# One kernel for attention with memory and two feed-forward stages: the order of the early attention steps, of the steps with tiles, and the engine that splits x

## The chip, the cores and the metric

The kernel runs on one core of one Trainium2 chip. The metric is the device time of one execution in microseconds (us). The engines are called as in the profile: PE is TensorE (PEld its weight loads), DVE is VectorE, ACT is ScalarE, POOL is GpSimd, SP is the engine that issues the DMAs.

## The reference

```python
def _attn_ref(q, k, v, M_prev, z_prev, beta):      # B, H, S, D = 4, 8, 576, 64
    scores = scale * np.matmul(q, k.transpose(0, 1, 3, 2))     # then a causal mask
    a = np.exp(scores - scores.max(-1, keepdims=True))
    a /= a.sum(-1, keepdims=True) + 1e-09
    local = np.matmul(a, v)
    q_p = np.where(q > 0, q, np.exp(q) - 1.0) + 1.0
    mem_out = (q_p @ M_prev) / (q_p @ z_prev + 1e-06)
    return g * mem_out + (1 - g) * local                       # g = sigmoid(beta) by head
def _moe_ref(x, w_in, w_out, g_ln):                # x: 2304 x 512, d_ff 1024
    h = x @ w_in
    solu = h * softmax(h)
    ln = (solu - mean) / np.sqrt(var + 1e-06) * g_ln
    return ln @ w_out
def _moe2_ref(x, w_gate, w_val, w_out):            # d_ff 1536
    return (sigmoid(x @ w_gate) * (x @ w_val)) @ w_out
```

## The kernel before, in words

All is fp32. The big products are made from high and low halves: an fp32r copy of a matrix (hi, an ACT cast) and what it leaves (lo, a subtraction), and three products hi*hi, hi*lo, lo*hi for each one.

Every engine has an order of its own, written out by hand, and the engines meet by semaphores. There are 16 pairs of heads (g=0 to 15) and 18 tiles of 128 tokens (t=0 to 17). In the early steps g=0 to 4 (`early_step`) there is attention alone. From g=5 (`step(g, t)`, t = g - 5) to g=16 a step holds the attention of pair g and the first feed-forward stage of tile t, and the output product of tile t-1. Then tiles 12 to 17 follow, and then the last stage.

Attention of one pair: PE makes the scores in four batches, `scores(g, 0)` to `scores(g, 3)`; the first three hold units 0 and 1, 2 and 3, 4 and 5, the last one unit 6. They are S0 to S3 in what follows. For each unit DVE takes the negated maximum and writes the scores out (`unit_max`, L905), and ACT makes the exponents and their sums (`exp_tile`, L588). DVE scales them by one over the sum (`normalize`, L929), in three batches. The units of S0, S1, S2 take turns in three banks of PSUM, so `scores(g, 2)` waits for the maximum of unit 2 and `scores(g, 3)` for that of unit 4:

```python
                elif n == 2:
                    pe.wait_ge(max_ok, NU * g + 3)
                else:
                    pe.wait_ge(max_ok, NU * g + 5)
```

In the next step PE turns P by seven groups of transposes (`turn_p`, L1349) through two banks, and each group is copied out to pT (`keep_pt`, L595 on ACT, L949 on DVE in steps with tiles); group n waits for copy n-2. In the step behind that one `weighted` makes the weighted values of P and v, with the memory's part turned in ahead (L1357, L1361): a main part over 512 tokens in o_bk and a tail over 64. ACT's `keep_x` copies both to xT (L602); tile by tile xT is the input of the feed-forward stage. `memory` (L1405) multiplies the features of q (`feature_relu`, `feature_exp` on ACT, `feature` on DVE, L913, called phi) with the memory, and DVE scales its result (`scale_memory`, L934 to L941).

Feed-forward of a tile: ACT casts x_hi (`moe_x`, L616), `split_x` makes x_lo (POOL, L546), PE makes 24 hidden products (`moe_hidden`, L1420), DVE and ACT make softmax and mean (`moe_max`, `moe_exp`, `moe_rows`, `moe_square`), POOL one over the deviation (`rstd`, L551), DVE the normalized rows (`moe_norm`, L1001). In the next step PE transposes them (`moe_transpose`, L1430), ACT casts ln_hi (`moe_ln`, L633), DVE makes ln_lo (`moe_ln_low`, L1008), and PE makes 24 output products (`moe_out`, L1444). The result is turned (`moe_out_t`, L1451) and stored back to xT (`moe_store_x`, L988).

x_hi of a tile is cast at the end of the step before, if all pairs that it needs are stored by then. The tiles for which this is not so are called OWN: t=0 and t=4. Their x_hi is cast in their own step, behind `keep_both`:

```python
        OWN = [t for t in range(PAIRS + 1 - M0) if HP * (((t + 1) * P - 1) // S + 1) > t + M0 - 2]
```

In the early steps the weights are split too, in between: w1 by `split_w1` (ACT L606, DVE L953), w2 by `split_w2` (ACT L611, DVE L958).

## Time and profile before

| | |
|---|---|
| runs | 845.44, 845.45, 846.02 us; median 845.45 |
| the profiled execution | 845.53 us, with a span of 843.5 us from the first to the last instruction |
| busy | PE 816.5, PEld 686.0, DVE 601.1, ACT 466.3, POOL 39.0 us |
| granted TensorE clock, mean | 0.995 |
| early steps g=1 to 4 | 11.73 to 64.17 us |
| steps with tiles, t=0 to 11 | 64.17 to 337.95 us |
| tiles 12 to 17, then the last stage | from 337.95 us |

Times in the rows are microseconds from the span's start. Matmuls are pipelined, and the busy time of PE takes in their overlap, so idle time of PE in the rows is a little less than the time lost: a row with "[0.40 <-DVE negmax L905]" says that PE had no instruction in flight for 0.40 us, and what ended that.

### The profile page before, as it was taken

Reading aid. Unit: us, or ns where it says so; the run is one execution under the profiler, and the core shown is the slowest. Engines: PE = TensorE matmul, PEld = TensorE weight load, DVE = VectorE, ACT = ScalarE, POOL = GpSimd, SP = SyncE. Lnnn points to the kernel's source line nnn. Section 1 sums busy time; section 2 is a strip of 40 time slices with the busy share of each in tenths; the row PEclk is TensorE's granted clock in tenths of the full one; section 3 lists DMA queues with packets and bytes.
Section 4 is the critical chain, followed back from the end, with each engine's and each line's share of the span. In section 5 each row is a group of like instructions: output and inputs, shape, how many; then the busy total and the mean of one; then the engine's idle time right before and its main releaser. Section 6 shows DMA issues by size and latency. Waiting matters only on the chain.

```text
span 843.5 us, 15401 instructions
## 1 busy us (share of the span) xinstructions
PE 816.5 (97%) x5704; PEld 686.0 (81%) x5704; DVE 601.1 (71%) x1447; ACT 466.3 (55%) x965; POOL 39.0 (5%) x47
## 2 busy tenths in 40 slices
PE   5888999999999999999999999999999999999997
PEld 3555777777777777878889999999999999999996
DVE  6988877777777775588565777687676678666653
ACT  6987666666566663364444444574444465444442
POOL 1000000000000001111000000000000000000000
PEclk8999999999999999999999999999999999999999
DMA  7353011111111000100224111103111113111002
GB/s 219 91 171 88 18 53 54 53 54 54 47 44 54 26 18 15 51 1 1 75 54 148 51 51 51 51 26 125 50 51 51 51 27 125 51 51 50 26 1 76
DMA packets 67034, 49.51 MB, mean 59 GB/s; under 512 B 9360, under 2 KB 57488, under 8 KB 66960
## 3 DMA queue, kind: packets, MB, share of 16 engines
q1 hardware_dynamic: 66960, 48.53, 19.3%
q8 instruction: 46, 0.75, 0.4%
q14 instruction: 28, 0.23, 0.1%
HBM read 43.79 MB, written 4.72 MB: 58 GB/s over the span
## 4 chain that ended last, share of the span: by engine, by line
PE 90%; DVE 5%; issue 2%; ACT 2%; SPq 1%; DMA 1%; POOL 0%; DVEq 0%; ACTq 0%
PE tt_bk L1554 10%; PE tt_bk L1552 10%; PE tt_bk L1553 10%; PE m_bk L1420 10%; PE s_bk L1444 7%; PE tt_bk L1349 5%; PE s_bk L1290 4%; PE o_bk L1357 4%; PE o_bk L1444 4%; PE s_bk L1604 3%; PE s_bk L1605 3%; PE s_bk L1603 3%; PE m_bk L1604 2%; PE m_bk L1605 2%; PE m_bk L1603 2%
## 5 line engine op out<-in xcount | busy, mean ns | idle before, releaser
L1554 PE MATMUL tt_bk<-xc_hi,wc_lo 128*128 128x384 f32 x476 | 160.0, 336 | 0.0
L1552 PE MATMUL tt_bk<-xc_hi,wc_hi 128*128 128x384 f32 x476 | 159.9, 336 | 0.0
L1553 PE MATMUL tt_bk<-xc_lo,wc_hi 128*128 128x384 f32 x476 | 159.8, 336 | 0.0
L588 ACT ACTIVATE p_nat<-p_nat,negmax 128x512 f32<-128x512 f32 (+2 forms) x144 | 83.0, 579 | 53.3 <-DVE negmax L905 53.3
L1133 DVE TENSOR_TENSOR wc_lo<-wc_raw,wc_hi 128x768 fp32r<-128x768 f32 x72 | 78.3, 1088 | 32.0 <-ACT wc_hi L653 32.0
L1552 PEld LDWEIGHTS tt_bk<-xc_hi,wc_hi 128*128 128x128 f32 x476 | 89.4, 188 | 6.1
L1553 PEld LDWEIGHTS tt_bk<-xc_lo,wc_hi 128*128 128x128 f32 x476 | 89.4, 188 | 6.1
L1554 PEld LDWEIGHTS tt_bk<-xc_hi,wc_lo 128*128 128x128 f32 x476 | 89.4, 188 | 0.0
L905 DVE CUSTOM_DVE_ANT_0 p_nat<-s_bk,mask 128x384 f32<-128x384 f32 (+2 forms) x124 | 54.9, 489 | 19.4 <-PE s_bk L1290 18.9
L653 ACT CAST wc_hi<-wc_raw 128x768 fp32r<-128x768 f32 x72 | 64.5, 946 | 3.1 <-DVE wc_raw L1127 3.1
L1349 PE MATMUL tt_bk<-ident,p_nat 128*128 128x128 f32 x400 | 56.6, 277 | 7.6 <-ACT pT L595 7.4
L595 ACT COPY pT<-tt_bk 128x512 f32<-128x512 f32 (+1 forms) x87 | 45.7, 552 | 31.9 <-PE tt_bk L1349 30.3
L1349 PEld LDWEIGHTS tt_bk<-ident,p_nat 128*128 128x128 f32 x400 | 46.7, 142 | 20.2 <-issue 13.4
L1290 PE MATMUL s_bk<-qkT 64*64 64x512 f32 (+3 forms) x496 | 47.7, 473 | 9.4 <-DMA qkT<-in_k 4.9
L1420 PE MATMUL m_bk<-w_hi,x_hi 128*128 128x512 f32 x120 | 50.5, 421 | 1.2 <-issue 1.2
L929 DVE TENSOR_SCALAR p_nat<-p_nat,c_loc 128x512 f32<-128x512 f32 (+2 forms) x144 | 50.1, 405 | 1.7
L690 ACT ACTIVATE gv_b<-tt_bk 128x384 f32<-128x384 f32 x34 | 16.7, 492 | 55.3 <-PE tt_bk L1554 55.3
L1420 PE MATMUL m_bk<-w_hi,x_lo 128*128 128x512 f32 x120 | 47.1, 392 | 0.0
L1420 PE MATMUL m_bk<-w_lo,x_hi 128*128 128x512 f32 x120 | 46.8, 390 | 0.0
L1149 DVE TENSOR_TENSOR c_u<-c_u,tt_bk 128x384 f32<-128x384 f32 x34 | 18.8, 553 | 37.4 <-ACT c_u L685 37.3
L700 ACT CAST gv_hia<-gv_a 128x384 fp32r<-128x384 f32 x36 | 18.5, 513 | 39.4 <-DVE gv_a L1164 39.4
L675 ACT ACTIVATE gv_a<-c_p 128x384 f32<-128x384 f32 x36 | 18.9, 526 | 36.3 <-DVE c_p L1144 36.3
(215 smaller groups left out, 1781.1 us busy)
## 6 DMA issues: line engine op xcount, KB each, us to landing
wc_raw<-in_moe_w_val SPq DMA_DIRECT2D x36, 256.0 KB, 3.0
wc_raw<-in_moe_w_gate SPq DMA_DIRECT2D x36, 256.0 KB, 3.4
qkT<-in_q SPq DMA_DIRECT2D x16, 288.0 KB, 2.8
qkT<-in_k SPq DMA_DIRECT2D x16, 288.0 KB, 3.2
v_raw<-in_v SPq DMA_DIRECT2D x16, 256.0 KB, 2.7
out<-o_sb SPq DMA_DIRECT2D x15, 256.0 KB, 2.5
w_raw<-in_moe_w_out SPq DMA_DIRECT2D x12, 256.0 KB, 4.5
turned<-in_k SPq DMA_DIRECT2D x32, 72.0 KB, 2.5
```

The lines of the kernel that those rows point to most:

```text
L588: nc.scalar.activation(p_tile(g, tile), p_tile(g, tile), ACT.Exp, bias=negmax[:, n:n + 1], scale=-1.0, accum_out=den[:, n:n + 1]).then_inc ...
L653: nc.scalar.copy(wc_hi[n % 2][:, k, :, :], wc_raw[n % NR][:, r, :, :]).then_inc(wc_hi_ok, 1)
L905: last = nc.vector.tensor_tensor_reduce(out=to, in0=s_tile(g, tile), in1=m, scale=-SCALE, scalar=3.0e38, op0=ALU.add, op1=ALU.min, accum_o ...
L929: nc.vector.tensor_scalar(p, p, c_loc[:, t:t + 1], None, ALU.mult).then_inc(p_ok, 1)
L1133: nc.vector.tensor_tensor(wc_lo[n % 2][:, k, :, :], wc_raw[n % NR][:, r, :, :], wc_hi[n % 2][:, k, :, :].bitcast(F32), ALU.subtract).then_ ...
L1290: last = mm(s_tile(g, tile)[c * D:c * D + D, :], qkT[r, g % 2, 0, a:a + D], qkT[r, g % 2, 1, 0:keys(tile)], start=True, stop=True, skip_gr ...
L1349: last = nc.tensor.transpose(bank[:, c * P:(c + 1) * P], p_nat[g % 2][:, p_at[tile] + j * P:p_at[tile] + (j + 1) * P], ident[:, :])
L1420: last = mm(h_banks(even)[:, n, :], x[:, b, :], w[:, b, c], start=m % (3 * DC) == 0, stop=m % (3 * DC) == 3 * DC - 1)
L1444: last = mm(y_bank(tail), ln[:, f * P:(f + 1) * P], w[:, f, :], start=m == 0, stop=m == 3 * FB - 1)
L1552: mm(o, hi[:, k, c, :], xc_hi[:, j, c, :], start=start and c == 0, stop=False, skip_group_check=True)
L1553: mm(o, hi[:, k, c, :], xc_lo[:, j, c, :], start=False, stop=False, skip_group_check=True)
L1554: last = mm(o, lo[:, k, c, :], xc_hi[:, j, c, :], start=False, stop=c == 1, skip_group_check=True)
```

## The change

1. In early steps PE makes the main part of the weighted values, then S1, then the tail; the memory's products stand behind transposes 2; S2 comes ahead of them. ACT takes copy n early: copy 0 between the two parts of `keep_x`, copies 1 and 2 ahead of the exponents of unit 2, and copies 3 to 6 ahead of exponents 4 to 8. DVE normalizes the first batch ahead of units 4 and 5, and takes unit 6 between the two parts of the memory's scaling; `feature` is last but for the splits of weights.
2. In steps with tiles PE makes S1 between the main part and the tail of the weighted values (t=1 excepted), and S2 always straight behind the memory's products; before it stood there for OWN tiles alone and else behind 12 of the hidden products. In the last of these steps (g=16) y is turned behind the weighted values, and ln ahead of them; ACT's and DVE's shares in ln_hi and ln_lo move ahead there too.
3. x_lo of tiles 0 to 12, but for t=4, is made on DVE and no longer on POOL: for t=0 behind units 2 and 3, for the others at the end of the step before.
4. In the first tile behind these steps ln_hi is cast ahead of `moe_square(t + 2)`, and ln_lo is made ahead of `moe_var(t + 2)`.

```diff
@@ gpsimd
-            def step(g):
-                if g >= M0:
-                    rstd(g - M0)
-                if g >= M0 - 1:
-                    split_x(g - M0 + 1)
-
-            for g in range(PAIRS + 1):
-                step(g)
+            def step(g, t):
+                if t and t in OWN:
+                    split_x(t)
+                rstd(t)
+
+            for g in range(M0, PAIRS + 1):
+                step(g, g - M0)
@@ scalar, early_step
                 exp_tile(g, 0)
                 exp_tile(g, 1)
                 if g > 1:
-                    keep_both(g - 2)
+                    keep_x(g - 2, 0)
                 if g:
                     keep_pt(g - 1, 0)
+                if g > 1:
+                    keep_x(g - 2, 1)
+                if g:
                     keep_pt(g - 1, 1)
-                for n in range(2, 6):
+                    keep_pt(g - 1, 2)
+                exp_tile(g, 2)
+                exp_tile(g, 3)
+                if g:
+                    for n in range(3, NF):
+                        keep_pt(g - 1, n)
+                for n in range(4, 6):
                     exp_tile(g, n)
-                if g:
-                    keep_pt(g - 1, 2)
-                    keep_pt(g - 1, 3)
                 for c in W1_HI_MID.get(g, ()):
                     split_w1(c)
                 for f in W2_HI_MID.get(g, ()):
                     split_w2(f)
                 exp_tile(g, 6)
                 exp_tile(g, 7)
-                if g:
-                    keep_pt(g - 1, 4)
-                    keep_pt(g - 1, 5)
-                    keep_pt(g - 1, 6)
@@ scalar, step
-                if t > 1 and g < PAIRS:
+                if t > 1:
                     moe_ln(t - 1)
                 keep_both(g - 2)
-                if t == 1 or g == PAIRS:
+                if t == 1:
                     moe_ln(t - 1)
@@ scalar, behind the steps
             moe_y(t, True)
+            moe_ln(t + 1)
             moe_square(t + 2)
             for i in range(t + 1, TILES):
                 even = (i - t) % 2 == 1
-                moe_ln(i)
+                if i > t + 1:
+                    moe_ln(i)
@@ vector
+            def split_x(t):
+                dve.wait_ge(x_hi_ok, t + 1)
+                nc.vector.tensor_tensor(x_lo[:, :, :], xT[:, :, bass.ds(t * P, P)],
+                                        x_hi[:, :, :].bitcast(F32), ALU.subtract).then_inc(x_lo_ok, 1)
@@ vector, early_step
                 unit_max(g, 2)
                 unit_max(g, 3)
+                normalize(g, 0)
+                unit_max(g, 4)
+                unit_max(g, 5)
                 if g:
                     scale_memory(g - 1, 0)
+                unit_max(g, 6)
+                if g:
                     scale_memory(g - 1, 1)
                     for c in W1_LO_MEM.get(g, ()):
                         split_w1(c)
-                unit_max(g, 4)
-                unit_max(g, 5)
                 feature(g)
...
-                unit_max(g, 6)
-                normalize(g, 0)
@@ vector, step
-                if t > 1 and g < PAIRS:
+                if t:
                     moe_ln_low(t - 1)
                 if t != 1:
                     normalize(g - 1, 2)
                 if g == PAIRS:
                     moe_store_x(t - 2)
-                if t == 1 or g == PAIRS:
-                    moe_ln_low(t - 1)
                 if g < PAIRS:
                     unit_max(g, 2)
                     unit_max(g, 3)
+                if t == 0:
+                    split_x(t)
...
                 moe_var(t)
                 moe_norm(t)
+                if t + 1 not in OWN:
+                    split_x(t + 1)
@@ vector, behind the steps
             moe_stats(t + 2)
-            low_xc(0, B21)
+            moe_ln_low(t + 1)
             moe_var(t + 2)
             moe_norm(t + 2, False)
+            low_xc(0, B21)
             for i in range(t + 1, TILES):
                 even = (i - t) % 2 == 1
-                moe_ln_low(i)
+                if i > t + 1:
+                    moe_ln_low(i)
@@ tensor, early_step (weighted is cut into weighted_main and weighted_tail)
                 scores(g, 0)
                 if g > 1:
-                    weighted(g - 2)
+                    weighted_main(g - 2)
                 scores(g, 1)
+                if g > 1:
+                    weighted_tail(g - 2)
                 if g:
                     turn_p(g - 1, 0)
                     turn_p(g - 1, 1)
-                    memory(g - 1, None)
                 scores(g, 2)
                 if g:
-                    for n in range(2, 5):
-                        turn_p(g - 1, n)
+                    turn_p(g - 1, 2)
+                    memory(g - 1, None)
+                    turn_p(g - 1, 3)
+                    turn_p(g - 1, 4)
                 scores(g, 3)
@@ tensor, step
                 if g < PAIRS:
                     scores(g, 0)
-                if g == PAIRS:
-                    pe.wait_ge(u_ok, t)
-                    weighted(g - 2)
-                if t > 1:
+                if 1 < t and g < PAIRS:
                     moe_out_t(t - 2)
...
+                weighted_main(g - 2)
+                if t == 1:
+                    weighted_tail(g - 2)
+                    moe_transpose(t - 1)
                 if g < PAIRS:
-                    weighted(g - 2)
-                if t == 1:
-                    moe_transpose(t - 1)
+                    wait(pe, yt_ok, t - 1)
+                    scores(g, 1)
+                if t != 1:
+                    weighted_tail(g - 2)
+                if g == PAIRS:
+                    moe_out_t(t - 2)
                 wait(pe, yt_ok, t - 1)
+                memory(g - 1, t)
                 if g < PAIRS:
-                    scores(g, 1)
-                memory(g - 1, t)
-                if t in OWN and g < PAIRS:
                     scores(g, 2)
                 pe.wait_ge(x_ok, 2 * (g - 1))
                 wait(pe, u_ok, t)
                 moe_hidden(t, 0, 12)
-                if t not in OWN and g < PAIRS:
-                    scores(g, 2)
```

## Rows read from the trace of the kernel before

**Rows 1.** Who PE waited for, whole span: us in total, times, longest.

```profile
PE tt_bk L1349 <- ACT pT L595: 7.4, 9, 1.2
...
PE s_bk L1290 <- DVE negmax L905: 2.4, 4, 0.9
...
PE tt_bk L1405 <- DVE ln_lo L1008: 1.5, 1, 1.5
```

**Rows 2.** Busy time by stretch: steps g=1 to 4, then t=3 and t=4.

```profile
11.73:24.38 12.65, 10.24 (x105) 5.70 (x106) 11.92 (x45) 10.96 (x31) 0.00 (x0) 0.73 0.64 210
24.38:37.97 13.59, 11.16 (x155) 7.17 (x155) 12.48 (x43) 12.75 (x33) 0.00 (x0) 1.00 0.30 87
37.97:50.79 12.82, 11.09 (x155) 7.15 (x155) 11.67 (x43) 10.70 (x29) 0.00 (x0) 1.00 0.33 98
50.79:64.17 13.38, 11.08 (x155) 7.17 (x154) 11.67 (x43) 11.54 (x31) 0.00 (x0) 1.00 0.77 232
...
131.05:154.21 23.16, 23.16 (x215) 17.33 (x214) 17.18 (x55) 14.13 (x35) 1.63 (x2) 1.00 0.17 47
154.21:177.68 23.47, 23.07 (x215) 17.43 (x215) 17.10 (x55) 15.33 (x36) 2.33 (x3) 1.00 0.18 49
```

**Rows 3.** Timeline of PE in t=3 (start, us, instruction): S2, first transpose.

```profile
141.52 0.66 PE L1290 MATMUL s_bk<-qkT 64*64 64x256 f32 x8
...
143.60 0.60 PE L1349 MATMUL tt_bk<-ident,p_nat 128*128 128x128 f32 x4
```

**Rows 4.** Timeline of DVE in t=3: unit 0, four normalized tiles, unit 2.

```profile
132.31 0.69 DVE L905 CUSTOM_DVE_ANT_0 p_nat<-s_bk,mask 128x512 f32<-128x512 f32 x1 [1.31 <-PE s_bk L1290]
...
134.54 1.14 DVE L929 TENSOR_SCALAR p_nat<-p_nat,c_loc 128x384 f32<-128x384 f32 x4
...
138.20 0.56 DVE L905 CUSTOM_DVE_ANT_0 p_nat<-s_bk,mask 128x384 f32<-128x384 f32 x1
```

**Rows 5.** Timeline of PE in t=4: S2, first hidden product, first transpose.

```profile
162.20 0.66 PE L1290 MATMUL s_bk<-qkT 64*64 64x256 f32 x8 [0.40 <-DVE negmax L905]
162.82 0.47 PE L1420 MATMUL m_bk<-w_hi,x_hi 128*128 128x512 f32 x1
...
167.01 0.93 PE L1349 MATMUL tt_bk<-ident,p_nat 128*128 128x128 f32 x7
```

**Rows 6.** Timelines of ACT and POOL in t=4: keep_x of the tail, x_hi, x_lo.

```profile
160.25 0.21 ACT L602 COPY xT<-m_bk 128x64 f32<-128x64 f32 x1
160.55 0.62 ACT L616 CAST x_hi<-xT 128x512 fp32r<-128x512 f32 x1
...
161.25 1.29 POOL L546 TENSOR_TENSOR x_lo<-xT,x_hi 128x512 fp32r<-128x512 f32 x1 [8.30 <-ACT x_hi L616]
```

**Rows 7.** Timelines of ACT in g=1 (w1_hi) and of DVE at g=2's start.

```profile
21.25 1.05 ACT L606 CAST w_hi<-xT 128x1024 fp32r<-128x1024 f32 x1
...
25.64 0.69 DVE L905 CUSTOM_DVE_ANT_0 p_nat<-s_bk,mask 128x512 f32<-128x512 f32 x1 [0.20 <-PE s_bk L1290]
```

**Rows 8.** Timelines of ACT and PE in t=0: x_hi, first hidden product.

```profile
70.53 0.62 ACT L616 CAST x_hi<-xT 128x512 fp32r<-128x512 f32 x1
...
72.69 0.47 PE L1420 MATMUL m_bk<-w_hi,x_hi 128*128 128x512 f32 x1 [1.17 <-issue]
```

**Rows 9.** Timeline of DVE in t=1: four normalized tiles.

```profile
88.06 2.16 DVE L929 TENSOR_SCALAR p_nat<-p_nat,c_loc 128x384 f32<-128x384 f32 x4
```

**Rows 10.** Timelines of PE and DVE in t=11: ln turned, memory's products, stored x.

```profile
320.62 1.04 PE L1430 MATMUL tt_bk<-ident,u_moe 128*128 128x128 f32 x8
323.27 0.81 PE L1405 MATMUL tt_bk<-mz,phi 64*64 64x66 f32 x40 [1.61 <-issue]
...
320.83 0.69 DVE L988 TENSOR_SCALAR xT<-s_bk 128x512 f32<-128x512 f32 x1 [0.29 <-PE s_bk L1451]
```

**Rows 11.** Timelines of DVE and PE at the first tile behind the steps: ln_lo, output product.

```profile
365.71 1.28 DVE L1008 TENSOR_TENSOR ln_lo<-tt_bk,ln_hi 128x512 fp32r<-128x512 f32 x2
...
367.05 0.50 PE L1444 MATMUL o_bk<-w_hi,ln_hi 128*128 128x512 f32 x1 [0.70 <-DVE ln_lo L1008]
```

More of the change, by code:

```diff
@@ L1362, in turn_memory, with weighted_main @@
                    is_transpose=True, skip_group_check=True)
-            def weighted(h):
+            def weighted_main(h):
                 wait(pe, x_ok, 2 * h)
@@ L1381, in weighted, with weighted_tail @@
                 last.then_inc(o_ready, 1)
+            def weighted_tail(h):
                 for j in range(ST):
@@ L1385, in weighted @@
                 last.then_inc(o_ready, 1)
+            def weighted(h):
+                weighted_main(h)
+                weighted_tail(h)
             def memory(g, t):
```

## The prediction

> **What bounds the kernel now.** I first read who TensorE (PE) waits for [rows 1, 8, 10]. Apart from some 7 us of start-up loads, its own idle time is about 16 us of 843.5, all before 370 us. It lies where the change works: 7.4 us at transposes of P that wait for ScalarE's (ACT's) copies, 2.4 us at scores that wait for VectorE's (DVE's) maxima, and the single waits of 1.6, 1.5 and 1.2 us at the memory's products of steps t=11 and t=1 and at the first hidden product of t=0. Behind 370 us PE works nearly without a gap, and the diff moves nothing there. So the sum is made in six places before that.
>
> Next, the work per step [rows 2]. In the early steps g=1 to 4 DVE is busy 11.92 of 12.65, 12.48 of 13.59, 11.67 of 12.82 and 11.67 of 13.38 us: it is nearly the bound, with 4.70 us without work in all. ACT has 10.96, 12.75, 10.70 and 11.54, PE some 11. In a step with tiles the picture turns over: t=3 lasts 23.16 us and PE is busy in all of it, DVE in 17.18. Such a step is PE's own work. It can only be shortened by taking work from PE, and can be lengthened by any new wait.
>
> **The third batch of scores, t=2 to 10.** S2 (units 4 and 5) waits until DVE has taken the maximum of unit 2. In t=3, the pattern of all but one of these steps, S2 stands in the middle of the hidden products, at 141.52, and never waits; the first transpose of P is at 143.60 [rows 3]. The step began at 131.05, so that is 12.55 us in. DVE is idle until the first scores come at 132.31 and then works without a gap: two maxima, the stored x, four normalized tiles, the low half of ln, three normalized tiles, and only then unit 2 from 138.20 to 138.90, 7.85 us in [rows 4]. The change leaves this order of DVE as it is for t=2 to 10. But it puts S2 straight behind the memory's products for all t. PE gets there some 7.6 us in (memory's products at 6.83 before, 0.7 long, and one more change of shape of 0.1, since the weighted tail now stands behind S1). So S2 waits.
>
> The trace has this very order already: t=4 is an OWN tile, and S2 stood behind the memory's products there. It waits 0.40 us for negmax, starts at 162.20, 7.99 us in, and the first transpose comes at 167.01, 12.80 us in [rows 5]. The order saves PE two changes of shape (S2 and 18 hidden products take 4.81 us together, against 5.03 for 12 products' tail, S2 and 6 more), but the wait costs more: +0.25 us to the transpose, +0.31 by the whole step, 23.47 against 23.16 [rows 2]. I take 0.28 for each of t=2, 3 and 5 to 10: **+2.2 us**. Moving S1 ahead of the weighted tail makes S1 ready 0.7 us sooner for DVE, but DVE comes to unit 2 only when its other work is done, and gains nothing by it. Bounds: if the wait were gone and the saved changes of shape alone were left, -0.15 per step, -1.2 us; if the full 0.40 came on top of an unchanged length, +3.2.
>
> **t=4 itself.** Its x_hi is cast behind keep_x of the tail, and that waits for the weighted tail, which now comes behind S1, 0.9 to 1.0 us later. In the trace keep_x of the tail starts at 160.25, x_hi at 160.55, the low half on GpSimd (POOL) at 161.25, 1.29 long to 162.54 [rows 6], and the first hidden product starts right behind S2 at 162.82 [rows 5]. There is no slack but 0.15. POOL keeps this one, so the hidden products start at about 163.7: **+0.85** (0 if something else gives, 1.0 at most).
>
> **Early steps.** The edits take DVE's wait for S1 (about 0.45 in each step) and PE's waits at the transposes away: copies 2 to 6 are taken before exponents they stood behind. With S2 and the maxima that follow moved up, DVE's idle time shrinks to 0.2 to 0.7 us in a step, waiting for S3. Against that ACT's splits of w1 and w2 now stand behind copies 3 to 6 and two exponents. For g=1 I follow the queue: unit 2's maximum ends at 18.3, S2 is at 18.5, copy 2 at 19.7 to 20.2, S3 at 21.1, transposes 5 and 6 at 21.8 and 22.4, copy 6 is done at 23.3, two exponents (0.99 the pair) at 24.3, and the cast of w1_hi block 0, which was at 21.25, ends at 25.25. DVE, which subtracts from it and started the next step at 25.64 [rows 7], is ready for it at 24.1, waits 1.3 us and starts the next step at 26.5: +0.9. g=2 has 0.7 us of idle DVE instead of 1.1 and next starts at 40.0 where it was 39.2; g=3 0.2 instead of 1.15, at 51.7 where it was 52.05; g=4 0.3 and another 0.9 of waiting for w2_hi, together 1.2 instead of 1.7, at 64.7 where it was 65.44. ACT has the same casts and exponents before x_hi of t=0 and less idle time, but its queue is longer behind copy 6; by the same count x_hi still ends at 71.1, as before. What comes there is the swap of engines: POOL took 1.6 us from the cast to the first hidden product at 72.69 [rows 8], DVE about 0.9 (a half of ln, 128x512, takes 0.6 [rows 11]). So hidden at 72.0: **-0.7**. DVE is blocked at split_x(0) for about 1.5 us, with memory scaling, unit 4 and unit 6 behind it; unit 4 is then ready at 2.6 us behind the first hidden product, S3 needs it at 2.9. That cover is 0.3 us thin; without it the step loses what is missing. Bounds: all of DVE's 4.70 us gone, -4.7; ACT's queue 1.5 us later at x_hi, +0.8.
>
> **t=1.** DVE now waits for x_hi and subtracts (about 1.2 us) ahead of normalizing. In the trace four such tiles took 2.16 us there, while POOL subtracted too, against 1.14 in t=3 [rows 4, 9]. That 1.0 comes back, so low ln is 0.2 later, and S2 behind the memory's products costs or saves 0.1: **-0.1**, within 0.4.
>
> The Trainium skill (SBUF — State Buffer, Who interferes with whom) says that the port pair which DVE and GpSimd share is an exclusive lock, held for a whole instruction. The trace agrees, with the 2.16 us. By that rule alone nine more subtractions off POOL should bring time; in t=2 to 10 they lie in DVE's 1.31 us of idle time before the first scores [rows 4], so by rule and row alike they bring nothing there.
>
> **t=11.** PE transposed y and then ln at 320.62, and the memory's products waited until 323.27 for low ln [rows 10]. Now ln's transpose comes first at 316.7 and low ln is ready at 319.8. But y's transpose, behind the weighted values, ends at 321.6, and the wait for yt_ok behind it takes DVE's store, 0.7 from transpose to start and 0.6 long [rows 10]: 322.5. **-0.75** (the full 1.6 at best).
>
> **The first steps behind.** PE waited 0.70 us at 367.05 for low ln, which DVE did at 365.71 [rows 11]. It now stands 2.2 us earlier on DVE, and the later maxima move up with it: **-0.75**; 0 if the next tile's low ln takes the wait back.
>
> GpSimd's freed queue, keep_x in two parts and qrelu's wait for phi (now at DVE's end, some 0.1 before ACT asks) I cost at nothing; if phi is late, ACT's exponent 8 is, and 0.2 a step go.
>
> **Sum.** 2.2 + 0.85 - 0.7 - 0.1 - 0.75 - 0.75 = +0.75. The profiled execution took 845.53, 2.0 beside its span, and the median is 845.45; both are one number here: **846.3 us**, no measurable change (within 0.2%, 843.8 to 847.1).
>
> **Rivals.** (A) The early steps run as smoothly as the edits allow: DVE's idle time goes nearly whole, since the casts of w1 and w2 are in time. From -0.7 to -4 there, 842.9 us: faster. It decides if the cast of w1_hi block 0 ends by about 24.1. For it: ACT and PE have slack in [rows 2]; against it: the casts' new place. (B) The wait at S2 doesn't come, DVE being ahead: -1.2 instead of +2.2, also about 842.9. Against it stands t=4's row. (C) The ends of ACT's and DVE's queues get late: x_hi(0) 1.5 us late, and split_x(0) holds unit 4 so that S3, the copies and the maxima of t=0 slip another 0.8. 848.6: slower. It decides once unit 4's maximum is over 0.3 us late. For it: DVE's queue was free to go on there and now stops. (D) The steps with tiles hide everything and the early gains end in the wait for x_hi: nothing changes, 845.5; that lies in my band.
>
> **Chances.** The forecast with D 0.62; A 0.13 and B 0.06 make faster 0.19; C 0.19. The range of 8 in 10 takes in most of A and of C: 843.0 to 848.3. The likeliest case by itself is 845.2 to 847.4.
>
> **What would show it.** S2 of every step 2 to 10 waits about 0.4 us for negmax, and each lasts about 23.45; t=4 about 24.3; the first hidden product of t=0 is near 72.0; DVE waits for w_hi near 24 to 25 us; the waits at t=11 and 367 shrink to about 1 and 0. If S2 does not wait, or DVE's idle time in g=1 to 4 falls below 1.5 us in all, I am wrong on the fast side; if unit 4 of t=0 is late, on the slow side.

## The result and the profile after

The changed kernel takes **854.86 us**, the median of five runs (852.29 to 856.19), against 845.45 before (845.37 to 846.02): ratio 1.0105, 95% interval 1.0094 to 1.0117. It is slower by 1.0%, clear of the noise, and far outside the forecast's range (843.0 to 848.3). The profiled execution took 854.86 us with a span of 853.1, against 845.53 and 843.5.

The first view is the busy time by stretch of the changed kernel. The stretches are those of [rows 2] with t=0 added (fifth row), each from one S0 to the next: g=1 to 4, t=0, t=3, t=4. A row has the stretch and its length, then the busy time (and number of instructions) of PE, PEld, DVE, ACT and POOL, then TensorE's granted clock as a share of full speed, the DMA engines' busy share and their GB/s.

```profile
11.10:24.29 13.19, 10.19 (x106) 6.31 (x106) 10.74 (x45) 8.55 (x24) 0.00 (x0) 0.74 0.59 198
24.29:38.02 13.73, 11.34 (x154) 7.25 (x155) 11.34 (x42) 12.94 (x33) 0.00 (x0) 1.00 0.28 81
38.02:51.09 13.07, 11.32 (x155) 7.27 (x155) 12.33 (x43) 11.19 (x31) 0.00 (x0) 1.00 0.29 85
51.09:68.16 17.07, 12.04 (x155) 7.87 (x155) 11.69 (x43) 10.40 (x30) 0.00 (x0) 0.95 0.67 196
68.16:91.28 23.12, 19.47 (x180) 12.77 (x179) 18.46 (x53) 18.78 (x48) 0.00 (x0) 0.89 0.28 78
139.31:162.74 23.43, 23.40 (x216) 17.40 (x215) 17.60 (x56) 14.23 (x35) 0.55 (x1) 1.00 0.16 46
162.74:187.31 24.57, 23.41 (x215) 17.39 (x214) 17.12 (x56) 15.23 (x36) 1.82 (x2) 1.00 0.16 47
```

Start with the lengths. g=4 takes 17.07 us where [rows 2] has 13.38, and t=0 takes 23.12 where it took 19.04 (64.17 to 83.21). These two stages hold 7.8 of the 9.6 us that the span grew. The steps with tiles are as forecast: 23.43 against 23.16 in t=3, 24.57 against 23.47 in t=4. The whole account against the kernel before, from PE's rows, with t=10 ending at its last product:

| stage | longer by, us | forecast |
|---|---|---|
| start, 11.10 for 11.73 | -0.6 | |
| g=1 to 3 | +0.9 | in the early steps' -0.7 |
| g=4 | +3.7 | in the early steps' -0.7 |
| t=0 | +4.1 | in the early steps' -0.7 |
| t=1 | 0.0 | -0.1 |
| eight steps t=2, 3, 5 to 10 | +2.0 | +2.2 |
| t=4 | +1.1 | +0.85 |
| t=11 | -0.6 | -0.75 |
| first tiles behind | 0.0 | -0.75 |
| last product to the span's end | -1.0 | not named |
| sum | +9.6 | +0.75 |

The start and g=1 are no firm numbers. In the eighteen other profiles g=1 begins between 10.80 and 11.93 us, and it lasts 11.75 to 13.56 us in four kernels that make it in the same way (w2_late, gap_filled, cast_late and hi_first, below). g=2 and g=3 agree to 0.01 us in these four.

The second view is who PE waited for, whole span, as in [rows 1]: us in total, times, longest.

```profile
PE s_bk L1303 <- DVE negmax L908: 7.9, 11, 1.5
PE s_bk L1335 <- DMA turned<-in_k: 4.5, 1, 4.5
...
PE m_bk L1439 <- issue: 1.9, 1, 1.9
...
PE m_bk L1439 <- POOL x_lo L546: 1.1, 1, 1.1
PE tt_bk L1362 <- ACT pT L594: 1.0, 2, 0.6
```

The waits for ACT's copies are gone, 1.0 us instead of 7.4, which is what the early edits do. In their place stand 7.9 us for maxima, where [rows 1] has 2.4, and a single wait of 4.5 us for a DMA that the kernel before doesn't have at all. The timeline of PE around g=4's end and t=0 shows where (start, us, instruction):

```profile
60.28 0.99 PE L1362 MATMUL tt_bk<-ident,p_nat 128*128 128x128 f32 x7
65.79 0.46 PE L1335 MATMUL s_bk<-qkT 64*64 64x288 f32 x2 [4.52 <-DMA turned<-in_k]
...
76.58 0.66 PE L1303 MATMUL s_bk<-qkT 64*64 64x256 f32 x8 [1.06 <-DVE negmax L908]
79.14 0.47 PE L1439 MATMUL m_bk<-w_hi,x_hi 128*128 128x512 f32 x1 [1.90 <-issue]
...
80.27 0.63 PE L1439 MATMUL m_bk<-w_lo,x_hi 128*128 128x512 f32 x1
80.69 0.63 PE L1439 MATMUL m_bk<-w_hi,x_lo 128*128 128x512 f32 x1
```

S3 of g=4 stands for 4.52 us until `turned`, the small turned copy of k that S3 multiplies with, has landed. Then t=0 waits twice, ahead of S2 and of the hidden products. The first hidden product is at 79.14, 10.98 us into the step; in [rows 8] it is at 72.69, 8.52 in. And from the fifth product on one follows the other after 0.43 us, not 0.23. The view by stretch shows TensorE's clock behind either wait:

```profile
65.79:70.00 4.21, 4.21 (x24) 1.92 (x25) 2.19 (x6) 2.32 (x7) 0.00 (x0) 0.59 0.42 105
...
79.14:83.65 4.51, 4.51 (x12) 3.20 (x12) 4.32 (x15) 3.08 (x12) 0.00 (x0) 0.62 0.00 0
```

Behind the stall seven transposes took 1.75 us for the 0.99 ahead of it, and S0 1.85 for 1.09 in the kernel before, and the first 12 hidden products took 4.51 us where the kernel before takes 2.91. By these rows about 3 of the 7.8 us are the lower clock (an estimate: 0.8 and 0.8 and 1.6).

Why `turned` is late is read from DVE's and SP's timelines, first DVE, then SP's issues, both of the changed kernel:

```profile
51.68 1.22 DVE L956 TENSOR_TENSOR w_lo<-xT,w_hi 128x1024 fp32r<-128x1024 f32 x1
```

```profile
52.92 4.58 SPq L476 DMA_DIRECT2D xT<-in_moe_w_out  x8
57.67 0.33 SPq L417 DMA_DIRECT2D qkT<-in_q  x1
58.04 0.43 SPq L420 DMA_DIRECT2D qkT<-in_k  x1
58.57 0.47 SPq L433 DMA_DIRECT2D turned<-in_q  x1
59.09 0.62 SPq L435 DMA_DIRECT2D turned<-in_k  x1
59.75 0.60 SPq L433 DMA_DIRECT2D turned<-in_q  x1
60.39 0.60 SPq L435 DMA_DIRECT2D turned<-in_k  x1
```

The last block of w1's low half is made at 51.68. SP waits for it (`w1_lo_ok`) before it loads w2, eight transfers of 256 KB whose issue takes 4.58 us, and `turned` for S3 stands behind them on SP's queue. In the kernel before the same rows read like this:

```profile
47.04 1.21 DVE L953 TENSOR_TENSOR w_lo<-xT,w_hi 128x1024 fp32r<-128x1024 f32 x1
```

```profile
48.28 3.66 SPq L476 DMA_DIRECT2D xT<-in_moe_w_out  x8
...
55.17 1.30 SPq L435 DMA_DIRECT2D turned<-in_k  x1
```

So the block is 4.6 us later, the w2 loads 4.6 later, and the last `turned` load is issued 5.2 later. The DMA view has 5.3 us from issue to landing for it, 6.0 in the kernel before. There it landed at 61.2, and S3 began at 61.29: the queue had no slack. PE's wait ends 14 us behind the block that caused it.

### The profile page after: what moved, and what is told of

It is laid out like the page before. It is cut to its first block, busy times and chain, and to the rows that moved or that the text cites. A ratio compares the mean times of both kernels' runs of the same rounds, so it can differ in the third digit from the quotient of the medians.

```text
span 853.1 us, 15409 instructions
## 1 busy us (share of the span) xinstructions
PE 822.5 (96%) x5704; PEld 688.9 (81%) x5704; DVE 604.5 (71%) x1459; ACT 467.2 (55%) x965; POOL 20.7 (2%) x35
## 4 chain that ended last, share of the span: by engine, by line
PE 89%; DVE 4%; ACT 3%; issue 2%; DMA 1%; SPq 1%; POOL 0%; DVEq 0%; ACTq 0%
PE tt_bk L1576 10%; PE tt_bk L1574 10%; PE tt_bk L1575 10%; PE m_bk L1439 10%; PE s_bk L1463 7%; PE tt_bk L1362 5%; PE o_bk L1463 4%; PE s_bk L1303 3%; PE o_bk L1370 3%; PE s_bk L1626 3%; PE s_bk L1627 3%; PE s_bk L1625 3%; PE m_bk L1626 2%; PE m_bk L1627 2%; PE s_bk L1439 2%; PE m_bk L1625 2%
## 5 line engine op out<-in xcount | busy, mean ns | idle before, releaser
L1303 PEld LDWEIGHTS s_bk<-qkT 64*64 64x64 f32 x496 | 15.6, 136 | 32.3 <-issue 15.5
```

Source lines behind the costliest of these rows:

```text
L1303: last = mm(s_tile(g, tile)[c * D:c * D + D, :], qkT[r, g % 2, 0, a:a + D], qkT[r, g % 2, 1, 0:keys(tile)], start=True, stop=True, skip_gr ...
```

## The experiments

Each median stands beside the kernel before on the same chip, which read 845.28 to 845.6 us in all five groups of runs. "The early steps" are g=1 to 4. All of them compute the reference. Diffs are shortened to the lines that tell the edit.

**early_back**: the changed kernel, `early_step` of ACT, DVE and PE as before.

```diff
-  early_step as changed (scalar, vector, tensor)
+  early_step as before
```

> The early steps g=0 to 4 as they were before, on PE, ACT and DVE; the steps with tiles and what follows as changed. Theory Q (a queue): the 9.4 us come almost all from the early steps, where DVE's low half of w1 block 3 came 4.6 us later, SP's loads of w2 and the small loads of turned q and k behind them went out 4.6 us later, and S3 of g=4 waited 4.5 us for turned; what is left is the 0.26 us in each of eight steps with tiles, 1.1 in t=4, less 0.8 in t=11 and some 0.5 in t=0: 847.3 us, 846.8 to 848. Rival R (the steps with tiles cost most, through the swap of engines or the granted clock): over 850.

846.07 us (ratio 1.0008, 0.9998 to 1.0017). Nearly the whole loss, 8.8 us, goes with the three early orders. It is below the expected 846.8 to 848: t=0 takes 18.34 us, 0.70 less than before, which is the gain that the prediction named for it.

**early_only**: the kernel before with the changed `early_step` of the three engines.

> The kernel before with the changed early steps alone. Theory Q: S3 of g=4 waits 4 to 5 us for turned, the clock falls behind it, and the time is 852.5 to 854. Rival R: within 2 us of 845.45.

852.36 us (1.0077, 1.0058 to 1.0095), with the wait for `turned` 3.7 us long. So 7.0 us of the loss need nothing of the rest of the change.

**w2_late** and **c3_early**: two ways to take `turned` from behind the late w2 loads.

```diff
 w2_late, SP
-               if g == 3: wait w1_lo_ok; load w2       # ahead of all loads of the next step
+               if g == 4: wait w1_lo_ok; load w2       # behind load_turned(4)
 c3_early, DVE in g=3
                 unit_max(g, 2); unit_max(g, 3)
+                split_w1(3)
...
                 scale_memory(g - 1, 1)
-                split_w1(3)
```

> The changed kernel, but SP issues the eight loads of w2 behind the loads of turned q and k for g=4 and no longer ahead of all loads of that step. Theory Q: the wait of 4.5 us at S3 of g=4 goes, and with it the stretches at a granted clock of 0.5 to 0.6 in the 15 us behind it (2.3 us): 847.5 to 849. Rival A (ACT's queue, whose casts of w2 stand behind copies 3 to 6, is what is late, and turned only shows it first): at most 1 us better than the changed kernel, or worse, since w2 lands later: 853.5 or more.

> The changed kernel, but DVE makes the low half of w1 block 3 straight behind unit 3's maximum in g=3, some 4 us sooner, as early as before; the queue of SP is as it was. Theory Q: w2 goes out at about 48.5 us, turned for g=4 at about 53.5, no wait at S3: 847.5 to 849. Rival A: 853 or more.

849.14 us (1.0046) and 850.97 us (1.0060). The wait at S3 is gone in both, and 3.9 to 5.7 us with it; both medians lie above the expected 847.5 to 849, c3_early's by 2 us. What is left against early_back, 3 to 5 us, is in t=0, which takes 24.2 us in both profiles against 18.34. Some of that is the edit's own: w2_late issues the load of v behind w2's, and PE waits 0.45 us for v at t=0's start. Most of it is the gap ahead of the hidden products. There the profile of w2_late shows, in windows from the memory's products to the first hidden product and then over the first 12 of them:

```profile
69.23:73.86 4.63, 1.48 (x53) 0.91 (x49) 3.40 (x15) 4.60 (x13) 0.00 (x0) 0.91 0.29 74
73.86:79.25 5.39, 5.39 (x13) 3.81 (x13) 4.57 (x15) 3.96 (x13) 0.00 (x0) 0.50 0.00 0
```

PE is busy 1.48 of 4.63 us, then works without a gap at a granted clock of 0.50, the lower of its two levels (1.2 GHz of 2.4). The 12 products take 5.39 us; in the kernel before they take 2.91 at a clock of 1.00.

**gap_filled** asks whether that clock follows from the gap. It is w2_late with 12 products in the gap whose result nobody uses.

```diff
   memory(g - 1, t)
+  if t == 0: fill(5)      # w1_hi by w1_hi into a bank that is free
   scores(g, 2)
+  if t == 0: fill(7)
```

> The changed kernel with the w2 loads behind turned(4) (849.14 us), and in t=0 TensorE makes products that nobody uses while it would wait: five of 128x128 by 128x512 behind the memory's products, seven behind S2. They fill the 1.25 and 1.9 us of waiting and delay nothing that was waited for. Theory 1 (the granted clock falls because of this gap): the 12 hidden products take 2.9 instead of 5.4 us and t=1 begins 2.5 us earlier, 846.5 us. Theory 2 (the low clock comes by itself): 849.1 us or a little more.

847.99 us (1.0027, 1.0016 to 1.0039). The same two windows:

```profile
69.67:74.63 4.96, 4.64 (x65) 3.01 (x61) 3.71 (x17) 4.93 (x14) 0.00 (x0) 1.00 0.26 70
74.63:77.54 2.91, 2.91 (x12) 2.14 (x13) 2.80 (x11) 1.49 (x7) 0.00 (x0) 1.00 0.00 0
```

The gap filled, the clock stays at 1.00 and the 12 products take 2.91 us. In the profiles PE's useless work saves 2.5 us at these products. The medians differ by 1.15, with overlapping intervals, and both kernels spread over 2.5 to 2.9 us, the slower executions at the lower mean clock (w2_late 848.21 us at 0.994 to 850.73 at 0.989, gap_filled 846.23 at 0.998 to 849.11 at 0.994); in which stretch the clock was low in the executions without a profile isn't known. The gap isn't enough by itself, though: early_only has 1.42 of 4.65 us busy there and a clock of 1.00 behind it. Its low clock is at the step's start, 0.78 over the 6.98 us ahead of that gap, behind the wait for `turned`.

**cast_late** (w2_late, two of the three w2 casts at g=4's end moved into t=0) and **hi_first** (w2_late, in t=0 the products that need x_hi alone first).

```diff
-        W2_HI_TILE, W2_HI_END = {5: (5, 6)}, {4: (2, 3, 4), 5: (7,)}
+        W2_HI_TILE, W2_HI_END = {5: (3, 4, 5, 6)}, {4: (2,), 5: (7,)}    # block numbers by step
```

> The changed kernel with the w2 loads behind turned(4), and of the three w2 casts that ScalarE makes at the end of g=4, two moved into t=0 behind the feature relu. Theory 1 (ScalarE's longer queue delays keep_x and x_hi of t=0, the gap of some 3 us at S2 and the first hidden product follows from it, and the granted clock falls to 1.2 GHz behind that gap): x_hi 1.2 us earlier, first hidden product at about 72.6 instead of 73.9, the first 12 hidden products 2.93 us instead of 5.39, t=1 begins at about 83.5 instead of 87.1, 845.6 us against 849.14. Theory 2 (VectorE's late maximum of unit 2 sets it; the casts don't matter): S2 still at 71.3 and the products still at 73.9, 849 us. Theory 3 (the gap shrinks, but the clock falls all the same): 847.9 us.

> The changed kernel with the w2 loads behind turned(4), and in t=0 the eight hidden products of the first bank that need x_hi alone are made first, the four with x_lo behind them. Nothing else moves. Theory 1 (the gap between S2 and the hidden products, then the clock): the first hidden product 1.1 us earlier, at 72.8, and with the shorter gap the 12 products take 2.93 to 4 us: 845.6 to 848 us against 849.14. Theory 2 (the low clock does not hang on this gap): -1.1 us alone, 848.0 us. Theory 3 (x_lo isn't what the hidden products wait for): no change, 849.1 us.

847.87 us (1.0029) and 847.27 us (1.0028). In cast_late the first hidden product is 2.72 us behind the memory's products instead of 4.63, and the clock stays at 1.00. But it gave some back: two late casts cost 0.9 us at the transposes, and the wait for v is 1.12 us here. Its median is the 847.9 of the third theory, but by luck: that theory has the clock fall. hi_first took 0.9 us off the gap, with the clock at 0.63 behind it; its profile is 1.9 us shorter in t=0 than w2_late's, and 1.3 shorter in g=1, which the edit doesn't touch.

**early_act_back** and **early_dve_back**: the changed kernel with one engine's early order taken back.

> The changed kernel with ScalarE's order of the early steps as before; PE's and VectorE's stay changed. Theory 1 (ScalarE's order isn't what made the stall at S3 of g=4; copies 2 to 6 late again cost PE its 0.9 us a step): the stall stays, 855 to 857 us. Theory 2 (ScalarE's order made x_hi of t=0 late and that is most of the loss): 851 us.

> The changed kernel with VectorE's order of the early steps as before; PE's and ScalarE's stay changed. Theory 1 (VectorE's order made w1_lo block 3 late, 51.7 instead of 47.0 us, and with it the w2 loads and turned): the stall of 4.5 us at S3 of g=4 is gone, 850.4 us or less against 854.86. Theory 2 (PE's or ScalarE's order made it late): 854 us.

848.74 us (1.0050, 1.0037 to 1.0064) and 861.64 us (1.0202). Neither came out as its first theory had it. Taking ACT's order back removes 6.1 us of the loss. DVE's old order beside the other two new ones is far worse, with 17.8 us of waits for maxima: PE's and ACT's new orders need DVE's. With ACT's order back the wait for `turned` is still 3.6 us, but t=0 takes 19.06 us, as long as before, and g=1 to 3 take 37.94 us where they took 39.06. The reason is in ACT's and DVE's timelines of t=0's start, here in one list. First the changed kernel, S0 at 68.16:

```profile
67.62 1.12 ACT L594 COPY pT<-tt_bk 128x512 f32<-128x512 f32 x2 [5.55 <-PE tt_bk L1362]
...
69.64 1.32 ACT L610 ACTIVATE w_hi<-xT,g_col 128x512 fp32r<-128x512 f32 x2
...
70.38 1.42 DVE L961 SCALAR_TENSOR_TENSOR w_lo<-xT,g_col,w_hi 128x512 fp32r<-128x512 f32 x2 [1.42 <-ACT w_hi L610]
71.71 0.69 DVE L908 CUSTOM_DVE_ANT_0 p_nat<-s_bk,mask 128x512 f32<-128x512 f32 x1
...
71.85 0.67 ACT L575 ACTIVATE qrelu<-qkT 128x576 f32<-128x576 f32 x1
...
77.70 0.62 ACT L615 CAST x_hi<-xT 128x512 fp32r<-128x512 f32 x1
```

and with ACT's order back, S0 at 66.00:

```profile
60.77 1.33 ACT L610 ACTIVATE w_hi<-xT,g_col 128x512 fp32r<-128x512 f32 x2 [0.90 <-DMA xT<-in_moe_w_out]
...
67.06 0.68 ACT L575 ACTIVATE qrelu<-qkT 128x576 f32<-128x576 f32 x1 [0.47 <-DMA qkT<-in_q]
...
68.20 0.68 DVE L906 CUSTOM_DVE_ANT_0 p_nat<-s_bk,mask 128x512 f32<-128x512 f32 x1
...
73.10 0.62 ACT L615 CAST x_hi<-xT 128x512 fp32r<-128x512 f32 x1
```

and in the kernel before, S0 at 64.17:

```profile
64.66 0.69 ACT L576 ACTIVATE qrelu<-qkT 128x576 f32<-128x576 f32 x1
```

In the new ACT order four exponents and the two w2 casts stand behind copies 3 to 6, which wait for PE's transposes, and these for S3. ACT stands idle for 5.55 us and then has that work left when t=0 begins. It comes to the relu of q 3.69 us behind S0, where it was 0.49, and from there to x_hi the work is the same, 5.85 us for 5.87. ACT isn't idle once between 67.62 and x_hi at 77.70: its own queue sets x_hi. w2_late, without the stall, has nearly the same (relu 3.59 us behind S0, x_hi 9.45), so this is the order and not the late `turned`. By another way DVE is late too: its low halves wait 1.42 us for the casts, and unit 0 of t=0 starts 3.55 us behind S0, not 2.2, and 1.27 in the kernel before. That delays unit 2, and so S2.

**early_mended** and **early_two**: can the early orders pay once this is mended? Both have the steps with tiles of order_back, below, the weighted values in one piece, and w1_lo block 3 early. early_mended keeps all three new orders, with the edits of cast_late and hi_first; early_two has ACT's old order.

> The kernel with the order back, but with the changed early steps, mended where they went wrong: w1_lo block 3 ahead in g=3, two w2 casts moved into t=0, in t=0 the products that need x_hi alone first, and the weighted values in one piece in the early steps too. Theory 1 (the changed order of the early steps gains nothing by itself; its waits for DVE and the casts only stand elsewhere): 843 to 844 us, no better than the kernel with the order back. Theory 2 (once the two late queues are mended its gain of 0.7 us or more shows): 842.3 us or less.

> The kernel with the order back (843.05 us), with PE's and VectorE's changed orders in the early steps (the weighted values in one piece), ScalarE's order of before, and w1_lo block 3 right behind unit 3 in g=3 so that the w2 loads are in time. Theory 1 (ScalarE's changed order made the loss; PE's and VectorE's alone gain, as S0 of g=1 to S0 of g=4 took 37.9 us against 39.1 before): 841 to 842 us. Theory 2 (the gain is given back at t=0 all the same): 843 us.

845.79 us (843.21 to 847.59) and 844.17 us (842.51 to 845.63), against 843.05 for order_back. In early_mended the early steps are shorter (S0 of g=1 to S0 of t=0: 50.9 us, 52.4 before; 1.0 of the 1.5 is g=1, which isn't firm), and it is given back in t=0, 21.1 us for 19.0: S2 waits 2.06 us there for a maximum, and the clock behind the gap is 0.62. In early_two t=0 is in order, 18.6 us, but g=3 took 14.95 us for 12.82, with a wait of 1.8 us for a maximum ahead of S2 and a mean granted clock of 0.89. Neither expectation of a gain came true. The runs also spread by 3 to 4 us, where order_back's lie within 1, and the slowest have the lowest mean clock (early_two 842.51 us at 0.998, 845.63 at 0.992).

**s2_back**, **s1_back** and **order_back** take the steps with tiles apart, all three with the early steps as before.

```diff
 s1_back, PE:  weighted_main(g - 2)
-              scores(g, 1); weighted_tail(g - 2)
+              weighted_tail(g - 2); scores(g, 1)
 s2_back, PE:  memory(g - 1, t)
-              scores(g, 2)
               moe_hidden(t, 0, 12)
+              scores(g, 2)          # OWN tiles keep theirs
 order_back = both
```

> The changed kernel with the early steps as before and, in the steps with tiles that are not OWN, S2 once more behind 12 hidden products. Only the place of S2 is taken back beside the early steps; S1 still parts the weighted values. Theory 1 (the wait of S2 for unit 2's maximum makes the longer steps): the eight steps t=2, 3, 5 to 10 fall from 23.42 to 23.16 us, 844.0 us in all against 846.07 with S2 ahead of the hidden products. Theory 2 (S1 between the two parts of the weighted values is what costs, by its changes of shape): the steps stay at 23.4, 846 us.

> As the kernel with S2 back, and S1 behind the weighted tail too, so that of the change only x_lo on VectorE, the order of t=11 and the first tile behind the steps are left. Theory 1: t=4 falls from 24.5 to 23.47 us, the other steps keep 23.16 or lose 0.05: 842.9 to 843.5 us, faster than before by 1.9 to 2.5 us. Theory 2 (what is left of the change gains nothing, its gains are given back behind 435 us): 845.3 us, the time before.

> The changed kernel with the early steps as before and, in the steps with tiles, S1 behind the weighted tail again; S2 stays straight behind the memory's products in every step. Theory 1 (the prediction's: S2 waits for unit 2's maximum, +0.28 us in each of eight steps): 845.3 us against the 843.05 of the kernel with both back. Theory 2 (S1 between the two parts is what costs; S2's place costs nothing): 843.0 us, steps of 23.1 to 23.2.

| | S2 | S1 | median, us | step t=3, us | step t=4, us |
|---|---|---|---|---|---|
| early_back | ahead | parts | 846.07 | 23.41 | 24.60 |
| s2_back | back | parts | 846.52 | 23.48 | 24.59 |
| s1_back | ahead | back | 845.11 | 23.50 | 23.48 |
| order_back | back | back | **843.05** | 23.17 | 23.47 |

Here is t=3 of s1_back, S2 straight behind the memory's products and S1 at its old place:

```profile
138.13 0.76 PE L1421 MATMUL tt_bk<-mz,phi 64*64 64x66 f32 x40
139.28 0.66 PE L1300 MATMUL s_bk<-qkT 64*64 64x256 f32 x8 [0.40 <-DVE negmax L906]
```

and the same of early_back, which differs in S1's place alone:

```profile
137.92 0.81 PE L1421 MATMUL tt_bk<-mz,phi 64*64 64x66 f32 x40
138.76 0.66 PE L1300 MATMUL s_bk<-qkT 64*64 64x256 f32 x8
```

In t=3 either move costs 0.31 to 0.33 us by itself and both together only 0.24. S2's move brings the forecast's wait of 0.40 us to the digit. S1's move brings changes of shape: from the main part to the next block 2.32 us pass instead of 2.21, for S1 1.02 instead of 0.91, for the tail 0.73 instead of 0.68, for the memory's products 0.74 instead of 0.69. With both, PE comes to S2 some 0.25 us later and DVE is nearly done. So in these eight steps taking one back gains nothing. By the medians S2 back alone costs 0.45 us and S1 back alone gains 1.0, with intervals that overlap, and both back gain 3.0. S1 back has its own gain in t=4: there the tail, x_hi and x_lo come early again and PE's wait of 1.13 us for x_lo is gone. order_back is faster than the kernel before: ratio 0.9973, 0.9962 to 0.9983.

**pool_back** and **tail_back** are order_back with x_lo on POOL again, and with the first tile behind the steps as before.

> The kernel with the order back (843.05 us) and x_lo on GpSimd again for every tile, so that only the order of t=11 and of the first tile behind the steps is left of the change. Theory 1 (the swap of engines is worth what PE waits less at the first hidden product of t=0, 1.34 instead of 1.84 us from S2 to the product, and nothing in the other steps): 843.6 us. Theory 2 (the span's last stretch, 4.27 us from the last product to the end before and 3.29 with the swap, hangs on the swap too): 844.6 us. Theory 3 (the 1.0 us that normalizing lost to GpSimd in t=1 counts as well): 1.0 us more than either.

> The kernel with the order back (843.05 us) and the first tile behind the steps as before: ln_hi behind the square, ln_lo behind the variance. Theory 1 (the wait taken away at the first tile, 0.95 us, comes back at the next one, 1.2 instead of 0.2): no change, 843.0 us within 0.3. Theory 2 (the prediction's: the wait is gone for good): 843.8 us.

844.61 us (0.9988) and 843.12 us (0.9969). The swap of engines is worth 1.56 us. 0.5 lie at t=0, S2 to the first hidden product in 1.34 instead of 1.84 us; t=1 is 0.2 longer with it (24.89 us for 24.69); 1.2 are at the span's very end (last section). The tail's new order is worth nothing: without it PE is idle for 0.72 us ahead of the first tile's output products and not at the next tile, with it not at the first and for 0.94 us at the next.

**order_hi**, order_back with hi_first's edit, is the same time.

> The kernel with the order back (843.05 us), and in t=0 the hidden products of the first bank that need x_hi alone ahead of those with x_lo. PE waits 0.7 us there for x_lo. Theory 1 (x_lo is what it waits for): 842.5 us. Theory 2 (the next wait takes it, the first transposes or unit 4): 843.0 us.

843.00 us (0.9966). The 0.7 us are gone from the first wait, and the four products with x_lo don't wait either. But S3 behind them now waits 0.34 us for unit 4's maximum, and the transposes 0.2 longer: t=0 takes 18.31 us instead of 18.51, and the time doesn't show it.

## Why the prediction was wrong

**The step that failed is the early steps' term, -0.7 us, where the rows show +8.7 (g=1 to t=0) and early_back 8.8.** It failed at two places that matter, both in queues that the sum had looked at only in part.

The first is SP's queue (the DMA issues). The edit on DVE puts unit 6 and the second memory scaling ahead of w1_lo block 3. The prediction costed DVE's end, followed DVE's work, and never asked who waits for that block: SP does, ahead of 2 MB of w2, and S3's `turned` is behind that. "GpSimd's freed queue, keep_x in two parts and qrelu's wait" were costed at nothing; SP's queue wasn't named. c3_early and w2_late, which take this wait alone away, are 3.9 and 5.7 us faster.

The second is "by the same count x_hi still ends at 71.1, as before". It began at 77.70, 9.54 us behind S0 where it was 6.36. The forecast did see that the w2 casts came later and priced it at 0.9 us of DVE (1.4 measured). It then took ACT to have "the same casts and exponents before x_hi" and left x_hi at its old time. The work is the same, but 3.2 us more of it are left behind S0, and ACT works through it without idle time. early_act_back bears it out: with ACT's order alone back, 6.1 us are gone and t=0 is as long as before. Rival C (queues' ends get late at x_hi, slower) named this mechanism, with x_hi 1.5 us late where it is 3.2, and without the clock. gap_filled shows the clock's part, 2.5 us in a profiled execution.

The count of the early steps themselves was off as well. It had DVE idle for 0.2 to 0.7 us in a step. In the rows by stretch DVE's busy time is 2.45, 2.39 and 0.74 us short of the length of g=1 to 3, and g=2 and g=3, which are firm, are 0.14 and 0.25 us longer than before instead of shorter.

The edits did do what the forecast said of them on PE: the waits at the transposes fell from 7.4 to 1.0 us, and DVE waited 1.1 us for w1_hi at 26.7, near the forecast 1.3. Whether the new orders save time in the early steps isn't shown: the profiles of early_act_back and early_mended have 1.1 us less over g=1 to 3 and 1.5 less over g=1 to 4, of which 0.6 and 1.0 are g=1, and neither kernel is faster in the end.

**The eight steps: size right (+2.0 for +2.2), reason right in part.** The wait of 0.40 at S2 came only with S1 at its old place. With S1 parting the weighted values, costed at one change of shape of 0.1, the shapes cost 0.31 and the wait falls to about 0.1. Two errors cancel: the sum came out by luck.

**t=4**: +1.1 for +0.85, the wait for x_lo on POOL, 1.1 us, as named; s1_back takes it away. **t=11**: -0.6 for -0.75, as named; the wait ahead of the memory's products fell from 1.61 to 0.78 us, now for DVE's store. **t=1**: nothing, for -0.1; S2's place saves 0.26 there (24.63 in s1_back, 24.89 in order_back) and the swap costs 0.2. **The first tile**: 0 for -0.75; the prediction's own bound ("0 if the next tile's low ln takes the wait back") is what happened, and tail_back shows it.

**The swap to DVE**: the 0.7 us at t=0 are 0.5 by pool_back, hidden in the changed kernel under the late x_hi. In t=1 DVE did get its 1.0 back, four normalized tiles in 1.14 us in order_back for 2.16 in pool_back, where GpSimd subtracts beside them. The Trainium skill (SBUF — State Buffer, Who interferes with whom) says that the port pair which DVE and GpSimd share is an exclusive lock; the traces agree, with these two numbers. But the time shows none of it: DVE's own subtraction takes 0.69 us ahead of them, and the step is 0.2 us longer in order_back.

What stays open: why early_only, with the same gap as w2_late, had no low clock behind it; how the 8.7 us split between the two queues, since they aren't additive (c3_early -3.9, ACT's order -6.1, all three orders -8.8); and how much of it is the clock in executions without a profile.

## What to carry to other kernels

When an instruction is moved on one engine, list who waits for each item that it now stands behind, down to the queue that issues the DMAs: 1.2 us of VectorE's work moved by 4.6 us held up a small load behind 2 MB and cost TensorE 4.5. Saving nearly 7 us of waits at the transposes was worth nothing, because what was moved behind the copies (exponents and casts of weights) was due sooner than the copies were. And test two moves of one change apart and together: here each cost 0.3 us a step alone, both cost 0.24, and leaving out only one, which moves the time by 1.0 us or less, would have hidden that leaving out both gives 3 us.

## What the runs showed of the hardware

TensorE's granted clock fell to 1.2 GHz behind idle time in the middle of kernels whose mean over the whole is 0.98 or more of 2.4: 0.50 for 5.39 us behind 4.63 us with 1.48 of work (w2_late), 1.00 when work of no use filled the same gap (gap_filled). There 3.15 us without work went with 2.5 us more behind them. The profiles of the other kernels, over the same two windows of t=0 (length of the gap, PE's work in it, clock of the first 12 hidden products): 2.72 us with 1.47, 1.00 (cast_late); 2.99 with 1.42, 1.00 (the kernel before); 3.43 with 1.37, 0.62 (early_mended); 3.71 with 1.48, 0.63 (hi_first); 4.43 with 1.47, 0.62 (the changed kernel); 4.93 with 1.47, 0.50 (c3_early); and, out of line with these, 4.65 with 1.42, 1.00 (early_only). These are one profiled execution each.

The span's end is 4.27 us behind the last product in the kernel before, 4.47 in pool_back and 4.38 in early_only, and 3.27 to 3.29 in the other sixteen kernels. The three are those with x_lo on GpSimd. The view of the DMAs of the last 3 us has a packet of an instruction queue in each of the three and in none of the sixteen; in pool_back it is

```profile
q14 instruction: 1, 0.01, 0.6%
```

So twelve subtractions fewer on GpSimd, all in the first half, took 1.0 to 1.2 us off the very end; pool_back and order_back differ by the swap alone, and by 1.2 us there. That this packet is what the end waits for is inferred, not shown.
